# The low halves of the mix weights: from VectorE to GpSimd, beside the fetch of their raw chunks

## The reference

```
attention: 8 heads of 64; chunks of 32 queries see 8 memory keys, 16 keys to the left, the chunk, 8 to the right
    a = exp(scores - max); a = a / (sum(a) + 1e-9); out = a @ v
mix:  x_prev = x shifted by one token
    xk = mu_k*x + (1-mu_k)*x_prev;  xr = mu_r*x + (1-mu_r)*x_prev
    k = max(xk @ w_k, 0);  v = (k*k) @ w_v;  r = sigmoid(xr @ w_r);  x = r*v
experts: each token goes to one of 8 experts (its own best one, or the one of the token before it,
    by a local gate);  out = p[e] * (max(x @ w1[e], 0) @ w2[e])
```

## Time and profile before

| | us |
|---|---|
| median of 3 runs | 498.62 |
| lowest, highest | 498.55, 500.6 |
| the profiled execution's own time | 499.68 |
| its span in the trace | 498.0 |

### The profile page before, as it was taken

One profiled execution on the slowest core, in us unless ns is written; L12 is line 12 of the kernel. 1 busy time (PEld: TensorE's weight loads), 2 busy tenths in 40 slices (PEclk: granted clock), 3 DMA queues, 4 the chain that ended last, 5 costly groups with the idle time before them and its releaser, 6 DMA issues.

```text
span 498.0 us, 9958 instructions
## 1 busy us (share of the span) xinstructions
PE 446.9 (90%) x3792; PEld 371.4 (75%) x3792; DVE 262.7 (53%) x592; ACT 222.1 (45%) x332; POOL 52.9 (11%) x70
## 2 busy tenths in 40 slices
PE   2775759999999999999999779999999999999991
PEld 2654549898898988988987557777777777777771
DVE  3576883434745447465584618223732274646851
ACT  2445652723537345372571036223712373727740
POOL 0001000000100101001001211111100011112110
PEclk9987578999999999999999879999999999999997
DMA  8889649753090540901901486410751176575610
GB/s 319 336 289 395 243 156 386 293 205 135 8 372 5 214 167 20 360 0 42 356 5 44 149 333 196 170 41 22 231 169 42 44 215 207 185 227 160 237 29 11
DMA packets 23728, 87.34 MB, mean 175 GB/s; under 512 B 3150, under 2 KB 3278, under 8 KB 23696
## 3 DMA queue, kind: packets, MB, share of 16 engines
q1 hardware_dynamic: 18048, 70.87, 39.1%
q0 software_dynamic: 5360, 16.04, 9.4%
q10 hardware_dynamic: 288, 0.02, 0.0%
HBM read 55.34 MB, written 32.62 MB: 177 GB/s over the span
## 4 chain that ended last, share of the span: by engine, by line
PE 72%; DMA 11%; DVE 7%; issue 5%; ACT 2%; POOLq 1%; POOL 0%; DVEq 0%; SPq 0%; ACTq 0%
PE PS L607 15%; PE PS L463 14%; PE PS L496 13%; PE PS L590 13%; PE PS L479 7%; DMA XR<-expert_rows 6%; PE PS L598 2%; PE PS L517 2%; PE PS L575 2%; DMA RAW<-wmix 2%; DMA QK<-tiles 1%; DMA VV<-tiles 1%; DVE EL L1084 1%; PE PS L507 1%; ACT WHI L703 1%
## 5 line engine op out<-in xcount | busy, mean ns | idle before, releaser
L1084 DVE TENSOR_TENSOR EL<-ERAW,EH 128x1024 fp32r<-128x1024 f32 x56 | 66.5, 1218 | 2.8 <-DVE META L1159 2.7
L781 ACT ACTIVATE EH<-ERAW 128x1024 fp32r<-128x1024 f32 x56 | 57.5, 1055 | 8.8 <-PE PS L607 8.8
L1152 DVE TENSOR_TENSOR HL<-PS,HH 128x512 fp32r<-128x512 f32 x32 | 22.1, 691 | 68.3 <-ACT HH L795 68.3
L607 PE MATMUL PS<-EH,HH 128*128 128x512 f32 x128 | 55.0, 430 | 3.3 <-issue 0.9
L463 PE MATMUL PS<-XHI,WHI 128*128 128x256 f32 x192 | 56.7, 295 | 0.9 <-issue 0.9
L590 PE MATMUL PS<-EH,XSH 128*128 128x512 f32 x128 | 53.3, 417 | 3.6 <-DVE EL L1084 3.6
L463 PE MATMUL PS<-XHI,WLO 128*128 128x256 f32 x192 | 55.2, 288 | 0.0
L463 PE MATMUL PS<-XLO,WHI 128*128 128x256 f32 x192 | 55.1, 287 | 0.0
L590 PE MATMUL PS<-EH,XSL 128*128 128x512 f32 x128 | 51.5, 402 | 0.0
L590 PE MATMUL PS<-EL,XSH 128*128 128x512 f32 x128 | 51.4, 402 | 0.0
L607 PE MATMUL PS<-EH,HL 128*128 128x512 f32 x128 | 50.9, 398 | 0.0
(11 more groups left out here) (147 smaller groups left out, 814.9 us busy)
## 6 DMA issues: line engine op xcount, KB each, us to landing
ERAW<-wexp SPq DMA_DIRECT2D x56, 512.0 KB, 5.0
expert_rows<-ZR SPq DMA_DIRECT2D x6, 4112.0 KB, 13.8
QK<-tiles SPq DMA_DIRECT2D x12, 768.0 KB, 6.4
VV<-tiles SPq DMA_DIRECT2D x12, 520.0 KB, 6.2
RAW<-wmix POOLq DMA_DIRECT2D x10, 512.0 KB, 6.0
XR<-expert_rows POOLq DMA_DIRECT2D x17, 257.0 KB, 4.5
CO<-consts SPq DMA_DIRECT2D x1, 340.0 KB, 4.8
rows_out<-OSB,OIDX POOLq DMA_INDIRECT x16, 5.3
```

The costliest lines, as they stand in the source:

```text
L607: last = nc.tensor.matmul(PS[4][:, :], x[:, f, :], ww[:, c:c + D], start=n == 0, stop=n == 23)
L781: nc.scalar.activation(expert_part(EH1, EH2, w, c), ERAW[c][:], ACT.Copy).then_inc(ehi_done, 1)
L1084: nc.vector.tensor_tensor(expert_part(EL1, EL2, w, c), ERAW[c][:], expert_part(EH1, EH2, w, c).bitcast(F32), ALU.subtract).then_inc(elo_do ...
L1152: nc.vector.tensor_tensor(HL[:, 4 * part:4 * part + 4, :].rearrange("p k n -> p (k n)"), PS[2 + part][:, :], HH[:, 4 * part:4 * part + 4, ...
```

## The change

The ten subtractions WLO = RAW - WHI leave VectorE's list and stand in GpSimd's, in between the transfers that GpSimd already issued. Waits and semaphores are the same ones; each transfer of a raw chunk from 2 on still waits for `wlo_done`, which GpSimd now raises itself.

```diff
@@ VectorE, attention(t)
-            def weight_lo(n):
-                dve.wait_ge(whi_done, n + 1)
-                c = mix_col(n)
-                nc.vector.tensor_tensor(WLO[:, c], RAW[n % 2][:], WHI[:, c].bitcast(F32),
-                                        ALU.subtract).then_inc(wlo_done, 1)
...
                 normed(t, u, t < 2)
-                if t >= 2:
-                    weight_lo(t - 2)
                 if t in (6, 7):
                     mix_full(0, t - 6, True)
...
@@ GpSimd
+            def raw_load(n):
+                if n < 2:
+                    pool.wait_ge(scores_done, n + 2)
+                else:
+                    pool.wait_ge(wlo_done, n - 1)
+                pool.dma_start(RAW[n % 2][:], wmix[:, n * CH1:(n + 1) * CH1]).then_inc(raw_loaded[n % 2], 16)
+
+            def weight_lo(n):
+                pool.wait_ge(whi_done, n + 1)
+                c = mix_col(n)
+                nc.gpsimd.tensor_tensor(WLO[:, c], RAW[n % 2][:], WHI[:, c].bitcast(F32),
+                                        ALU.subtract).then_inc(wlo_done, 1)
+
+            for n in range(2):
+                raw_load(n)
             for n in range(N1):
-                if n >= 2:
-                    pool.wait_ge(wlo_done, n - 1)
-                else:
-                    pool.wait_ge(scores_done, n + 2)
-                pool.dma_start(RAW[n % 2][:], wmix[:, n * CH1:(n + 1) * CH1]).then_inc(raw_loaded[n % 2], 16)
+                weight_lo(n)
+                if n + 2 < N1:
+                    raw_load(n + 2)
```

## The result

The changed kernel took 503.69 us in the median of 8 runs (500.14 to 505.01), the kernel before 499.12 us in 8 runs beside it (497.35 to 501.28). The ratio is 1.0082, with a 95% interval of 1.0053 to 1.0111: slower by 4.1 us, 2.6 to 5.5 (the two medians differ by 4.6). The forecast was 503.0, in a range of 498.0 to 506.5, and 4.4 us above 498.62, the median of before that it went by. Every ratio here leaves out slow runs, those over 1.5% above the fastest of their kernel: none of these 16, but 11 of 23 runs of the kernel before in the last series.

The account below looks back on a forecast made before the run. DMA was taken as the heaviest load to 46.6 us, VectorE to 68 us, TensorE from the mix at 74.75 us. Ring +0.3 and holds +0.9, +0.9, +1.4, +1.0 made +4.5 us: forecast 503.0 us, range 498.0 to 506.5.

Parts of the forecast that it names:

- The price of the subtraction: Each WLO on GpSimd: 2.45 us, twice VectorE's time, between bounds of 1.22 and 3.7 us.
- The hold: VectorE's XF (tiles 6, 7) and XLO (tiles 8, 9) wait until GpSimd's WLO ends: +0.9, +0.9, +1.4, +1.0 us.
- The ring: Raw-buffer refills: chunks 3 and 4 issued later, idle time won at tile 5 paid back, WHI of chunk 4 +0.3 us.
- The end of the stage: Last attention tile: chunk 9 lands at 76.6 us, its WHI ends before XT of the last tile, hidden by 0.7 us.
- The instruction marked ISA: Ahead of GpSimd's first subtraction: covered, with 8.9 us to hide it, even for a first call of some 6 us.
- the last WLO and SyncE's fills: After attention: last WLO ends near 80.3 us instead of 74.2, expert-row fills come 6 us later; all covered.
- The sum: Whole kernel: +4.5 us on the profiled 499.68 gives 504.2; from the runs' median 498.62, 503.1, stated as 503.0.
- Rival 1: XF and XLO not held, the ring eats the gain: +0.5 us at the mix's start, 499.1 us; chance 0.32.
- Rival 3: Subtraction dearer on GpSimd, at 3.7 us: holds grow and chunk 4 lands later, near +10.7 us, 509; chance 0.13.
- rival 2: GpSimd costs near 1.22 us, nothing held: 497.9 us, up to -3 if QK's transfers start earlier; chance 0.07.

Follow-up runs that it names:

- after_again: The changed kernel, unaltered, run once more for its own time and a second trace; ratio 1.0080 to the kernel before.
- before_again: The kernel before, unaltered, run once more for a second trace; 501.51 us in a single run.
- after: The changed kernel in its first profile, all ten subtractions on GpSimd; 503.69 us, ratio 1.0082 to the kernel before.
- b_dve67: The changed kernel with the subtractions of chunks 6 and 7 back on VectorE; ratio 1.0043 to the kernel before.
- e_memset: The changed kernel with GpSimd filling zeros in place of the subtractions of chunks 4 to 7; 500.15 us in a single run.
- f_copy: The changed kernel with two one-input GpSimd copies in place of each subtraction of chunks 4 to 7; 486.5 us in a single run, not comparable.
- t3_wait: The changed kernel with a third raw buffer, GpSimd's subtractions of chunks 4 to 7 waiting until XF or XLO is done; ratio 0.9959 to the kernel before.

## Why the prediction was right

- **The price of the subtraction**: 2.45 us predicted, 2.36 measured. That a ratio from two small fills of the earlier trace rows led so near was luck: on the large tile a fill takes 0.95 us and the subtraction 2.36. With the ratio of 1.96 for a two-input operation that the Trainium skill (GPSIMD Engine Reference, Performance versus the Vector engine) has, the estimate would have been 2.4; the trace agrees, at 2.356 / 1.225 = 1.92.
- **The hold**, on which the forecast rested and which no row of before could show, is there at all four places, and VectorE is held at no other. As sums: +0.9, +0.9, +1.4 and +1.0 us predicted, +0.60, +0.60, +1.13 and +0.67 measured (after_again against before_again in the table, both at a granted clock of 0.50 from 60 us on), 3.0 us instead of 4.2. The term was too large for two reasons: the subtraction is 0.1 us shorter, and the held instruction has begun when the hold ends, so that XLO ends 1.08 us behind it, where I had put its whole 1.22, and XF 1.47, where I had put 1.67. The Trainium skill (SBUF — State Buffer, Who interferes with whom) has VectorE with two inputs in SBUF contend with a GpSimd instruction that reads SBUF, and not with one that only writes. after, b_dve67, e_memset and f_copy together agree, with 2.48 us for XLO, 2.34 for XF, and 1.23 and 2.11 for XLO again, beside GpSimd.
- **The ring**: +0.3 predicted. Over seven traces with two buffers and GpSimd subtracting chunks 0 to 3 the ring's mean is 23.8 us, over the two of the kernel before 23.4: +0.4, inside a spread of 1.6, so that its size is not shown. What it consists of was also as put: the 1.77 us of idle time at tile 5 are gone, and a wait of 1.43 us for chunk 4 has come. What I undervalued is how much there was to win: I counted 1.77 us at tile 5 only, and the kernels with three buffers show another 0.9 to 1.7 us between WHI of chunk 1 and of chunk 3.
- **The end of the stage**: chunk 9 was to be hidden by 0.7 us. In the first trace WHI waited 0.59 us for it and XT still waited 1.34 us for TensorE: hidden. The instruction marked ISA cost nothing: GpSimd's first WLO starts 0.09 us behind WHI's end. Of the last WLO and SyncE's fills no cost is to be seen, within the spread of 4 us behind the mix's start.
- **The sum**: 3.0 + 0.4 is 3.4 us, against 4.1 (2.6 to 5.5) by the ratio and 79.90 - 76.55 = 3.35 us by the two later traces, after_again and before_again. That 3.4 and 3.35 agree to 0.1 is again partly chance, since the ring alone spreads by more. The predicted 4.4 is inside the interval, and 1 us above what the rows add up to; that the whole came out at 503.69 against 503.0, though the holds were put 1.2 us too high, owes something to luck.
- **Rival 1** (no hold) is out by the rows of XLO. Its second half was true: the ring does eat what VectorE gains. **Rival 3** (a dearer subtraction) and **rival 2** (faster) are out by 2.36 us and by the ratio; but rival 2's ground, that a lighter VectorE speeds up the stage, comes true once the third buffer is there.

What stays open: why the ring's length varies by up to 1.5 us from trace to trace of one kernel. The later start of the first trace after is another matter: there TensorE waited longer for the load of QK of tile 2, whose scores began at 15.50 us instead of 13.73, and the first WHI came 1.56 us later.

## What to carry to other kernels

Before an elementwise operation goes to GpSimd, list VectorE's instructions with two operands in SBUF that can run at that time: each that starts while GpSimd reads waits for its end, and the profile books this as a longer instruction, not as idle time. An operation that frees the buffers of a ring adds the slower engine's extra time to each refill: here the gain came through only with a third buffer. And where a change is worth less than the spread of a run, compare distances between instructions in the changed stage.

## What the runs showed of the hardware

- GpSimd takes 2.36 us for a two-input fp32 subtraction of 128 x 1024, 1.03 to 1.05 us for a one-input copy of that size, and 0.95 us for a fill. Three subtractions back to back in t3_wait take 6.98 us, 2.33 each. The copy is as fast as ScalarE's (WHI: 1.04 us); it is the second input that costs.
- A hold between VectorE and GpSimd works both ways: whichever starts second waits (XLO 2.48 us, WLO 2.80 us).
- Transfers that GpSimd issued during VectorE's long two-input operations took 0.56 us to issue in the changed kernel (at 51.85 and 65.79 us), the median of all ten there.
- The kernel before ran its last attention tile at a granted clock of 1.00 (2.4 GHz) in one trace and of 0.50 (1.2 GHz) in the other; the end of the stage differs by 0.83 us between these two runs of one program.
